# Casting the next network's input during the last wide chunk, and its second weight matrix after it: a Trainium2 kernel

## The reference

```python
def _moe_ref(x, w_ch1, w_ch2):
    ...
    u = x + mixed
    un = (u - mu) / np.sqrt(var + 1e-06)
    ch = np.maximum(un @ w_ch1, 0.0) @ w_ch2
    return (u + ch).astype(np.float32)

def _moe2_ref(x, w_in, conv_w, w_out):
    B, S, D_ff = (*x.shape[:2], w_in.shape[1])      # 4, 576, 1024
    h = np.maximum(x @ w_in, 0.0)                   # 512 -> 1024
    hp = ...                                        # h with one zero row before and behind
    conv_out = np.zeros_like(h)
    for k in range(K):                              # K = 3
        conv_out += conv_w[k][None, None, :] * hp[:, k:k + S, :]
    gate = 1.0 / (1.0 + np.exp(-conv_out))
    return (h * gate @ w_out).astype(np.float32)    # 1024 -> 512
```

## Time and profile before

| | before |
|---|---|
| median of 3 runs | 844.83 us (844.43 to 846.24) |
| the profiled execution | 844.43 us |
| its span, first to last instruction | 842.6 us |
| PE busy | 823.0 us (98%) |
| DVE busy | 431.3 us (51%) |
| ACT busy | 301.7 us (36%) |
| POOL busy | 263.4 us (31%) |

### The profile page before, as it was taken

One profiled execution on the slowest core, in us unless ns is written; L12 is line 12 of the kernel. 1 busy time (PEld: TensorE's weight loads), 2 busy tenths in 40 slices (PEclk: granted clock), 3 DMA queues, 4 the chain that ended last, 5 costly groups with the idle time before them and its releaser, 6 DMA issues.

```text
span 842.6 us, 15876 instructions
## 1 busy us (share of the span) xinstructions
PE 823.0 (98%) x6420; PEld 739.4 (88%) x6420; DVE 431.3 (51%) x812; ACT 301.7 (36%) x879; POOL 263.4 (31%) x342
## 2 busy tenths in 40 slices
PE   8998999999999999999999999999999999999998
PEld 8677799998999899999998788888889889898986
DVE  5766745556443434564753131222227867477563
ACT  4664553446133341332322222212124343335332
POOL 2896774268220555160000405051510500000000
PEclk9999999999999999999999999999999999999999
DMA  9952432134101103300033101010100010010101
GB/s 210 250 125 72 100 75 59 40 88 114 45 15 41 56 17 125 101 26 26 26 129 129 63 0 63 1 62 1 63 1 1 1 51 1 9 55 1 51 1 62
DMA packets 79490, 49.64 MB, mean 59 GB/s; under 512 B 60225, under 2 KB 69209, under 8 KB 79418
## 3 DMA queue, kind: packets, MB, share of 16 engines
q1 hardware_dynamic: 77706, 44.37, 19.3%
q10 hardware_dynamic: 1712, 4.26, 1.4%
HBM read 39.18 MB, written 9.45 MB: 58 GB/s over the span
## 4 chain that ended last, share of the span: by engine, by line
PE 89%; DVE 4%; POOL 2%; DMA 2%; ACT 1%; issue 1%; SPq 1%; DVEq 0%
PE banks L806 14%; PE banks L823 13%; PE banks L941 12%; PE banks L958 11%; PE banks L915 10%; PE banks L900 10%; PE banks L764 4%; PE banks L737 3%; PE banks L711 2%; PE banks L640 2%; PE banks L626 2%; PE banks L673 1%; PE banks L659 1%; POOL w1aL L1635 1%; PE banks L685 1%; PE banks L696 1%
## 5 line engine op out<-in xcount | busy, mean ns | idle before, releaser
L806 PE MATMUL banks<-unH,w1aH 128*128 128x256 f32 x288 | 85.0, 295 | 0.4 <-DVE hL L1332 0.4
L823 PE MATMUL banks<-hH,w2aH 128*128 128x256 f32 x288 | 84.4, 293 | 0.0
L1464 DVE SCALAR_TENSOR_TENSOR hw<-banks,hw 128x512 fp32r<-128x512 f32 x32 | 22.1, 691 | 120.3 <-ACT hw L1125 120.3
L1673 POOL TENSOR_TENSOR accw<-accw,rstd_bc 128x512 f32<-128x512 f32 (+1 forms) x20 | 23.7, 1216 | 191.6 <-DVE accw L1348 88.4
L823 PE MATMUL banks<-hL,w2aH 128*128 128x256 f32 x288 | 81.4, 283 | 0.0
L806 PE MATMUL banks<-unL,w1aH 128*128 128x256 f32 x288 | 81.4, 283 | 0.0
L806 PE MATMUL banks<-unH,w1aL 128*128 128x256 f32 x288 | 81.4, 282 | 0.0
L823 PE MATMUL banks<-hH,w2aL 128*128 128x256 f32 x288 | 81.3, 282 | 0.0
L900 PE MATMUL banks<-unw,w1bH 128*128 128x512 f32 x256 | 78.9, 389 | 1.0 <-DVE unw L1459 1.0
L915 PE MATMUL banks<-hw,w2bH 128*128 128x512 f32 x256 | 79.0, 390 | 0.8 <-DVE hw L1464 0.8
L1056 ACT ACTIVATE hH<-banks 128x256 fp32r<-128x256 f32 x80 | 30.7, 383 | 134.5 <-PE banks L806 134.5
(11 more groups left out here) (192 smaller groups left out, 2157.7 us busy)
## 6 DMA issues: line engine op xcount, KB each, us to landing
qk_in<-in_q SPq DMA_DIRECT2D x32, 144.0 KB, 2.8
qk_in<-in_k SPq DMA_DIRECT2D x32, 144.0 KB, 2.9
v_grp<-in_v SPq DMA_DIRECT2D x16, 288.0 KB
acc_dram<-astage SPq DMA_DIRECT2D x9, 512.0 KB, 2.6
accw<-acc_dram SPq DMA_DIRECT2D x9, 512.0 KB, 4.8
out<-ostage SPq DMA_DIRECT2D x16, 256.0 KB, 2.7
v_win<-in_v SPq DMA_DIRECT2D x32, 122.5 KB
w2araw<-in_moe_w_ch SPq DMA_DIRECT2D x4, 512.0 KB, 7.5
```

Of the source, the lines that this page charges most:

```text
L806: last = nc.tensor.matmul(bank[0][:, 0:CT], w[wp][:, t, P * m:P * m + P], (unH, unL)[xp][:, t, :], start=(t == 0 and i == 0), stop=(t == P ...
L823: last = nc.tensor.matmul(bank[1 + d // 2][:, CT * (d % 2):CT * (d % 2) + CT], w[wp][:, m, P * d:P * d + P], (hH, hL)[xp][:, m % 2, :], st ...
```

## The change

Four things move, all at the handover from the mixing network to the gated one. The instructions stay the same in number and shape; their places in memory and in the engines' orders change.

1. **Memory.** x2H and x2L move behind w2b, where the statistics of the normalization (cent, part, total) were before. hw and accw move into the place of woH: hw takes the first half of it, accw the second.
2. **x2 of batch 0.** ACT casts its four parts after relu_wide of tiles 1 to 4 of the last wide chunk, and DVE subtracts after split_wide of the same tiles, where both stood behind the whole chunk. The cast of a quarter of wi moves from behind tile 2 to behind tile 5 in every wide chunk.
3. **wo.** Since hw and accw now lie in woH, no quarter of it can be cast while a wide chunk runs. On ACT, quarter 0 comes right behind the last wide chunk, quarter 1 in batch 0 behind the two copies of tile 1, quarters 2 and 3 behind those of tiles 4 and 5. Quarters 0 and 1 wait for the last contract_wide, 2 and 3 for the last finish.
4. **POOL.** The four low_wo come after the wide chunks: two before the last finish, two behind it. The wait of the last finish for tile 3 of batch 0 is gone. On PE contract2(0, m) waits for the quarter of woL that it reads. SP's first load into accw waits for the last sums of the first half (acc_full) in place of the variances (var_full).

```diff
--- before.py
+++ after.py
@@ -349,11 +349,8 @@
         w1bH, w1bL, w1braw = split_pair("w1b", [P, PB, FH])
         w2bH, w2bL, w2braw = split_pair("w2b", [P, MA, D])
         stat_at = top[0]
-
-        top[0] = stat_at + 2048
-        hw = sb("hw", [P, 2, 2, WT], F32R)
-        accw = sb("accw", [P, PB, WT])
-        accw_at = top[0] - 4 * PB * WT
+        x2H = sb("x2H", [P, PB, S], F32R)
+        x2L = sb("x2L", [P, PB, S], F32R)
         hpad = [sb("hpad0", [P, S + 2])]
         rstd_bc = sb("rstd_bc", [P, WT])
 
@@ -370,11 +367,14 @@
 
         top[0] = wa_at
         wiH, wiL, wiraw = split_pair("wi", [P, PB, FF2])
+        wo_at = top[0]
         woH, woL, woraw = split_pair("wo", [P, M2, D])
 
+        top[0] = wo_at
+        hw = sb("hw", [P, 2, 2, WT], F32R)
+        accw = sb("accw", [P, PB, WT])
+
         top[0] = scratch_at
-        x2H = sb("x2H", [P, PB, S], F32R)
-        x2L = sb("x2L", [P, PB, S], F32R)
         hpad.append(sb("hpad1", [P, S + 2]))
         conv = [sb(f"conv{u}", [P, 2, S]) for u in range(2)]
         gate = [sb(f"gate{u}", [P, S]) for u in range(2)]
@@ -388,7 +388,7 @@
         remH = sb("remH", [P, M2, 2 * REM], F32R)
         remL = sb("remL", [P, M2, 2 * REM], F32R)
         ostage = sb("ostage", [P, FULL + 1, D])
-        assert top[0] <= accw_at
+        assert top[0] <= stat_at
 
         banks = [ctx.enter_context(nc.psum_tensor(f"banks{i}", [P, 2, 512], F32)) for i in range(4)]
         bank = [banks[i // 2][:, i % 2, :] for i in range(8)]
@@ -574,7 +574,7 @@
                     store_rstd()
 
             sp.wait_ge(a_stored, 16 * NCH)
-            sp.wait_ge(var_full, B)
+            sp.wait_ge(acc_full, 2 * NCH)
             sp.dma_start(accw[:, :, 0:CT], acc_d[0]).then_inc(b_loaded, 16)
             sp.wait_ge(rstd_stored, 16)
             sp.dma_start(rstd_bc[:, 0:CT], rstd_d[0:CT].partition_broadcast(P)).then_inc(bc_loaded, 16)
@@ -945,8 +945,9 @@
 
             def contract2(b, m):
                 pe.wait_ge(hgL_ok, M2 * b + m + 1)
+                if b == 0:
+                    pe.wait_ge(woL_ok, m // 2 + 1)
                 if b == 0 and m == 0:
-                    pe.wait_ge(woL_ok, PB)
                     pe.wait_ge(accw_kept, PB * NW)
                 for tt in o_tiles(b):
                     if m == 0 and tt % 2:
@@ -1124,6 +1125,13 @@
                 act.wait_ge(hw_full, MA * w + m + 1)
                 nc.scalar.activation(hw[:, m % 2, 0, :], wide_bank(m), ACT.Relu).then_inc(hwH_ok, 1)
 
+            def round_wo(i):
+                if i < 2:
+                    act.wait_ge(accw_full, PB * NW)
+                else:
+                    act.wait_ge(x_fin, NW + 1)
+                nc.scalar.copy(wo_part(woH)[:, i], wo_part(woraw)[:, i]).then_inc(woH_ok, 1)
+
             for t in range(PB):
                 round_wide(0, t)
             for w in range(NW):
@@ -1132,19 +1140,19 @@
                         for t in range(PB - 1):
                             round_wide(w + 1, t)
                     relu_wide(w, m)
-                    if m == 2:
+                    if w == NW - 1 and m in (1, 2, 3, 4):
+                        if m == 1:
+                            act.wait_ge(x_fin, 2)
+                            act.wait_ge(var_full, B)
+                        round_x2(0, m - 1)
+                    if m == 5:
                         act.wait_ge(wi_in, 16)
                         nc.scalar.copy(wiH[:, w], wiraw[:, w]).then_inc(wiH_ok, 1)
-                    if m == 4:
-                        act.wait_ge(wo_in, 16)
-                        nc.scalar.copy(wo_part(woH)[:, w], wo_part(woraw)[:, w]).then_inc(woH_ok, 1)
                 if w + 1 < NW:
                     round_wide(w + 1, PB - 1)
 
-            act.wait_ge(x_fin, 2)
-            act.wait_ge(hw_full, MA * NW)
-            for t in range(PB):
-                round_x2(0, t)
+            act.wait_ge(wo_in, 16)
+            round_wo(0)
 
             def batch(b, last_one):
                 for m in range(M2 + 2):
@@ -1155,6 +1163,8 @@
                             at_least(act, hg_ok, M2 * b + max(m - 1, 0))
                             nc.scalar.activation(hpad[m % 2][:, 1 + HS * c:1 + HS * c + HS], bank[5 + g % 3][:, 0:HS],
                                                  ACT.Relu).then_inc(h2_relu, 1)
+                    if b == 0 and m in (1, 4, 5):
+                        round_wo((1, 4, 5).index(m) + 1)
                     if 1 <= m <= M2:
                         act.wait_ge(c_step, 3 * (M2 * b + m))
                         nc.scalar.activation(gate[(m - 1) % 2][:], conv[(m - 1) % 2][:, 0, :], ACT.Sigmoid).then_inc(gated, 1)
@@ -1481,10 +1491,10 @@
                     split_wide(w, m)
                     if m == 0 and w:
                         add_wide(w - 1)
+                    if w == NW - 1 and 1 <= m <= PB:
+                        low_x2(0, m - 1)
                 if w + 1 < NW:
                     low_wide(w + 1, PB - 1)
-            for t in range(PB):
-                low_x2(0, t)
             add_wide(NW - 1)
 
             dve.wait_ge(accw_kept, PB * NW)
@@ -1686,12 +1696,15 @@
                                         ALU.subtract).then_inc(woL_ok, 1)
 
             finish(0, slice(0, CT), slice(0, CT))
-            for w in range(NW):
+            for w in range(NW - 1):
                 low_wi(w)
-                low_wo(w)
-                if w == NW - 1:
-                    pool.wait_ge(hgL_ok, PB)
                 finish(w + 1, slice(0, WT), wide(w))
+            low_wi(NW - 1)
+            low_wo(0)
+            low_wo(1)
+            finish(NW, slice(0, WT), wide(NW - 1))
+            low_wo(2)
+            low_wo(3)
 
 
 # ---- launch: one core; inputs and outputs as the reference has them ----
```

## The result

| | before | changed |
|---|---|---|
| median, same chip | 844.93 us (844.43 to 846.24, 4 runs) | 852.1 us (850.95 to 853.48, 4 runs) |
| ratio | 1 | 1.0083, 95% interval 1.0062 to 1.0103 |
| the profiled execution, its span | 844.43 us, 842.6 us | 852.5 us, 850.7 us |

The change makes the kernel slower by 7.2 us in this comparison. The forecast was 850.2 us, 5.8 us slower.

A forecast was written before the change was run, and what follows sets the result against it. PE, busy 98% of the span, was taken as the bound. To the profiled 844.43 us came +4.8 (6.9 of lateness less 2.1 of waits saved) and +1.0 for the clock: 850.2 us, range 846.0 to 854.0.

The forecast's parts named there:

- What was said to win nothing: Wide chunks and first expand2: moving x2 and the wi cast gains zero, since PE did not wait there.
- The collision: Batch 0: POOL's low_wo(1) and last finish slow DVE's gated work; first remL at 655.9, contract2(0, 0) 6.9 us late.
- The ratio of 2.4: DVE's slowdown beside POOL, from 4.29 to 10.34 us in the earlier trace; it turns 5.45 us of work into 13.1.
- the ring: DVE's repeating gated-network work per tile, which feeds PE; a round and next first step take 4.29 us alone.
- PE's lateness: Batch 0: about 4 us idle ahead of half unit 9, 1 to 2 ahead of 7, a rest at contract2(0, 0).
- ACT's cast of quarter 1: Batch 0, tile 1: the wo cast delays table load and first sigmoid by 1.05 us, costing DVE's gated work 0.8.
- the old waits: Batch 0: contract2's two waits for remL in the kernel before, 2.1 us in all, vanish.
- The clock: Batch 0: a PE wait of 4 us makes the granted clock fall, costing 1.0 us, bounds 0 and 1.7.
- the weak collision: Batch 0: DVE runs only 1.7 times slower, first remL 3.1 us late; 845.4 to 847 us, chance 0.13.
- the faster case: Batch 0: DVE keeps pace beside POOL and only the 2.1 us of waits go; 842.3 us, chance 0.05.
- the steady clock: Batch 0: idle pieces shorter than 2.6 us, so the granted clock stays up; 849.2 us, chance 0.12.
- The full block: Batch 0: DVE pays POOL's nine instructions in full, first remL 10.9 us late; some 854 to 855 us, chance 0.10.

The follow-up runs named there:

- the memsets: Changed kernel with the last finish replaced by eight POOL memsets of about the same length, which read nothing from memory: 846.38 us beside 845.04, ratio 0.9998.
- full clock: Changed kernel with PE's idle time ahead of half units 7 and 9 filled with unread matmuls: 851.37 us beside 845.50, ratio 1.0063; stretch 54.80 us.
- the spread finish: Kernel before with the last finish cut into four pairs placed where DVE waits: 842.82 us beside 845.04 (0.9986), again 844.42 beside 846.29 (0.9975).
- the early finish: Kernel before with the last finish on POOL no longer waiting for tile 3 of batch 0: 846.23 us beside 845.04, ratio 1.0022.

## Why the prediction was right

**What was said to win nothing won nothing.** PE went into the first expand2 without a gap, before and after, with x2 moved and with x2 put back. From the first expand_wide to the first expand2 the changed kernel took no longer than before, so the move of the wi cast cost nothing either.

**The collision.** This was the step that carried the sum, and it held: POOL started low_wo(1) 8.0 us behind the first expand2 (forecast 8.0) and ended the finish 23.7 us behind it (forecast 22.8 to 23.8). The first remL ended 22.6 us behind, forecast 22.7. The ratio of 2.4 came back: one round of the ring plus the next first step took 10.28 us, against 10.34 and 4.29 in the earlier trace rows; the busy times of that stretch (length, PE, PEld, DVE, ACT, POOL, PEclk, DMA) of the changed kernel:

```profile
650.30:660.58 10.28, 7.00 (x40) 6.64 (x40) 10.17 (x8) 3.12 (x8) 9.92 (x7) 0.83 0.01 2
```

DVE and POOL are both busy all through it. The memsets show that the cause was named rightly.

**PE's lateness.** Forecast: waits ahead of half units 7 and 9 and at contract2(0, 0), about 7 us, none behind. Measured: 2.27 and 3.27 us ahead of these two half units, contract2(0, 0) 6.8 us late at full clock, and no wait behind it. The wait at half unit 9 was shorter than the 4 us forecast, the one at 7 longer; at contract2(0, 0) it was 0.55 us at full clock and nothing in the first profile, where the low clock had made PE later still.

**Three terms were mis-sized.** Two of them cancelled, and that is luck. From the start of low_wo(1) to the end of the first remL, DVE worked for 13.8 us (14.6 us less the wait of 0.84), where 2.4 times its own work had given 13.1. Line 1517 took 2.84 us beside low_wo(1), 3.5 times its own 0.82. And ACT's cast of quarter 1 was priced at 0.8 us on the ring but cost nothing by itself: the sigmoid ended at 646.4, while line 1517, blocked by low_wo(1), ended only at 647.7. What delayed the first hg, by 2.0 us, was that block. So the first remL came as forecast, 0.7 us too little in one term standing against 0.8 too much in the other.

The third is the old waits. I had counted their idle time of 2.1 us and left out the restarts; the spread finish shows that they cost 2.65 us (50.49 - 47.84). Because of it the handover at full clock costs 54.80 - 50.49 = 4.3 us, where 4.8 was forecast.

**The clock.** It fell in all three profiles of the changed kernel, and cost 0.4, 1.0 and 1.8 us; forecast 1.0 with bounds 0 and 1.7. The kernel before, the early finish and the memsets kept it at 1.00 through the stretch, with waits of at most 2.44 us.

**The sum.** The three profiles of the changed kernel give 4.7, 5.3 and 6.1 us for the handover; 5.8 was forecast. The 7.2 us of the first comparison are above that. The ratios of the three comparisons, 1.0083, 1.0052 and 1.0097, have intervals of 0.2 to 0.3% on either side; their mean, 0.8%, is some 6.5 us. I attribute 4.7 to 6.1 us of it to the handover. The rest is within the spread of executions ahead of the handover; no row of the profiles puts it on the change.

The rivals: the weak collision and the faster case are out with the ratio of 2.4, the steady clock with the falls in all three profiles. The full block is out in its size: contract2(0, 0) came 6.8 us late, not 10.9. For the single instruction it is nearer than that. Beside a POOL instruction of 2.39 us alone, line 1517 took 2.84; a full block would be 3.2. Beside one of 1.26 us it took 1.7 where a full block would be 2.1.

## What to carry over

Before work is moved to an engine or a time where it "runs beside" something, look up what else reads memory there: here POOL had been idle for 43 us, and its work made the ring on DVE 2.4 times as long as soon as it met it. Place such work by the waits of the other engine, in pieces that fit into them; the same finish cost PE 2.65 us in one piece and nothing in four. And judge a handover by its own stretch in the profile, with the granted clock beside it. Two profiles of the spread finish agreed to 0.01 us there, while the medians of whole runs move by one or two. Where the clock fell, three profiles of one kernel still differed by 1.3 us.

## What the runs showed of the hardware

- A DVE instruction with two inputs in SBUF that meets a reading POOL instruction took its own time plus POOL's, less 0.2 to 0.4 us. Line 1514 or 1517: 0.82 alone, 1.74 beside POOL instructions of 1.26 us, 2.84 beside one of 2.39. The shorter ones beside 1.26 us: 0.75 became 1.81, 0.69 became 1.75, 0.22 became 1.29.
- Line 1501, a tensor_scalar of 576 columns, took 1.54 to 1.97 us where POOL's reads ran all through it, but 0.52 beside POOL's memsets, its time alone.
- Idle times of PE did not decide alone whether the clock fell: behind 2.27 us it stayed at 1.00 in one profile of the changed kernel and fell in another, and in two with the same waits, 2.27 and 3.27 us, the low stretch cost 0.4 and 1.8 us.
